# Two token mixings and the order of transposes at the start of a fused mixing and two-MLP kernel

## The reference

```
# x: (2, 4096, 192); weight_gen: (2, 4096, 8 heads, 7 taps); both MLPs: 192 -> 2048 -> 192
w = softmax(weight_gen, over the 7 taps)
mix[b, s, head, :] = sum over k of w[b, s, head, k] * x_pad[b, s + k, head, :]   # 24 features a head, 6 rows of zeros ahead
t = mix.reshape(8192, 192)
h = t @ moe_w_in;  t = max(0.01 * h, h) @ moe_w_out                      # MLP 1, leaky ReLU
h = t @ moe2_w_in; out = where(h > 0, h, exp(min(h, 0)) - 1) @ moe2_w_out  # MLP 2, ELU
```

## Time and profile before

| | us |
|---|---|
| median of 3 runs | 1184.88 |
| lowest and highest of them | 1182.89 and 1187.18 |
| the profiled execution | 1186.27 |
| span of its trace | 1183.6 |
| PE busy in the span | 1160.1 |
| DVE, ACT and POOL busy | 661.4, 750.1 and 422.3 |

### The profile page before, as it was taken

How to read it: one execution, slowest core, us unless ns; L and a number is a source line. 1 busy time by engine, 2 the same in 40 slices (tenths; PEclk the granted TensorE clock), 3 DMA queues, 4 the chain that set the end, 5 groups by cost and what they waited for, 6 DMA issues and landing times.

```text
span 1183.6 us, 22757 instructions
## 1 busy us (share of the span) xinstructions
PE 1160.1 (98%) x9808; PEld 927.1 (78%) x9808; DVE 661.4 (56%) x690; ACT 750.1 (63%) x846; POOL 422.3 (36%) x409
## 2 busy tenths in 40 slices
PE   6899999999999999999999999999999999999998
PEld 4777887878878777887878878778787878878776
DVE  6766736456474554636446374564736556364554
ACT  3566757567575665657666575665757657575665
POOL 5727531707135090541806226080440806200000
PEclk9999999999999999999999999999999999999999
DMA  5312021020101101021020110201121020110000
GB/s 171 115 50 67 25 78 28 28 79 22 57 28 47 59 28 52 28 78 28 28 66 27 65 28 28 79 28 52 28 78 28 28 65 22 34 28 28 15 28 27
DMA packets 44724, 55.45 MB, mean 47 GB/s; under 512 B 4117, under 2 KB 32915, under 8 KB 44625
## 3 DMA queue, kind: packets, MB, share of 16 engines
q1 hardware_dynamic: 44624, 54.01, 14.8%
HBM read 36.29 MB, written 17.69 MB: 46 GB/s over the span
## 4 chain that ended last, share of the span: by engine, by line
PE 87%; DVE 4%; ACT 3%; POOL 3%; issue 2%; DMA 1%; SPq 0%; POOLq 0%
PE y_a_rows L617 27%; PE hidden L549 27%; PE y_b L610 19%; PE hidden L553 9%; PE hidden L578 5%; DVE hid_lo L1125 2%; DVE act L1100 2%; ACT hid_hi L915 1%; ACT act L899 1%; POOL mix L325 1%; POOL prod L313 1%; DMA wk<-in_weight_gen_dram 0%; ACT ya L873 0%; DMA xw<-in_x_dram 0%; POOL prod L337 0%
## 5 line engine op out<-in xcount | busy, mean ns | idle before, releaser
L617 PE MATMUL y_a_rows<-hid_hi,dn 64*128 64x512 f32 x2048 | 574.7, 392 | 0.0
L610 PE MATMUL y_b<-hid_hi,dn 64*128 64x512 f32 x1024 | 401.5, 392 | 0.5 <-PE y_b L610 0.2
L610 PE MATMUL y_b<-hid_lo,dn 64*128 64x512 f32 x1024 | 400.9, 392 | 0.0
L617 PEld LDWEIGHTS y_a_rows<-hid_hi,dn 64*128 64x128 f32 x2048 | 332.5, 185 | 44.8
L617 PE MATMUL y_a_rows<-hid_lo,dn 64*128 64x512 f32 x1024 | 359.2, 391 | 0.0
L1125 DVE TENSOR_TENSOR hid_lo<-hidden,hid_hi 128x1024 fp32r<-128x1024 f32 x128 | 156.5, 1222 | 231.4 <-ACT hid_hi L915 231.2
L1125 DVE TENSOR_TENSOR hid_lo<-act,hid_hi 128x1024 fp32r<-128x1024 f32 x127 | 169.8, 1337 | 178.4 <-ACT hid_hi L915 176.7
L897 ACT ACTIVATE hidden<-hidden 128x1024 f32<-128x1024 f32 x127 | 128.2, 1009 | 184.5 <-PE hidden L553 184.5
L313 POOL TENSOR_TENSOR mix<-xw,wk 128x384 f32<-128x384 f32 x30 | 39.0, 1301 | 571.8 <-DVE wk L1041 566.3
L899 ACT ACTIVATE act<-hidden 128x1024 f32<-128x1024 f32 x127 | 130.3, 1026 | 141.7 <-PE hidden L553 135.3
L549 PE MATMUL hidden<-in_a_hi,up_a_hi 64*128 64x512 f32 x1020 | 205.5, 399 | 7.2 <-DVE act L1100 3.4
(11 more groups left out here) (104 smaller groups left out, 1189.4 us busy)
## 6 DMA issues: line engine op xcount, KB each, us to landing
xw<-in_x_dram SPq DMA_DIRECT2D x14, 960.0 KB
raw_b<-squares_out SPq DMA_DIRECT2D x60, 96.0 KB, 2.2
out_dram<-staged SPq DMA_DIRECT2D x15, 384.0 KB, 2.5
squares_in<-prod SPq DMA_DIRECT2D x56, 96.0 KB, 2.0
squares_out<-ya SPq DMA_DIRECT2D x15, 256.0 KB, 2.0
raw_a<-squares_in SPq DMA_DIRECT2D x14, 256.0 KB, 2.8
raw_d<-in_moe_w_out_dram SPq DMA_DIRECT2D x8, 384.0 KB, 3.4
raw_a<-in_moe_w_in_dram SPq DMA_DIRECT2D x8, 256.0 KB, 3.7
```

The source lines that it names most:

```text
L610: return nc.tensor.matmul(y_b[:, :], dn[m][rows, f, P:2 * P], v[rows, s % HB, HALF[i]], start=start, stop=stop)
L617: return nc.tensor.matmul(bank[:, :], dn[m][rows, f, first:first + P], v[rows, s % HB, HALF[i]], start=(f == 0 and n == 0), stop=(f == FT ...
```

## The change

**First mixing.** Two more buffers, `term4` and `term5`, are laid into the part of `act` that the first phases don't use. Products 4 and 5 go to them and product 6 to `staged_rows`, so that no product waits for PE, and `s_termu` is gone. On DVE the first part of chunk 1's softmax (`softmax_a(1)`) moves from ahead of the mixing to between the two parts of chunk 0's input; on ACT its exponential moves behind chunk 0's input.

**Warm-up.** The two matmuls of L789 are gone.

**Chunk 1's input.** Part 0 is turned behind step 7 of phase 0. Phase 1 begins with the down work of step 5, then part 1 is turned, then the down work of step 6; up of step 8 follows in both parts. Step 9 takes the down work of step 7, and step 10 is up alone. ACT and DVE split part 0 behind their work on step 7.

**Layout.** `wk1`, the softmax weight buffer of odd chunks (896 bytes a partition), is allocated last, so that every buffer between moves by its size.

```diff
@@ -94,7 +94,7 @@
         xw = sb("xw", [P, PAD + J, D], f32)
-        wk = [sb(f"wk{n}", [P, J * H, TAPS], f32) for n in (0, 1)]
+        wk = [sb("wk0", [P, J * H, TAPS], f32)]
         wmax = sb("wmax", [P, J * H], f32)
         wsum = sb("wsum", [P, J * H], f32)
         wrec = sb("wrec", [P, J * H], f32)
@@ -122,7 +122,10 @@
         ya = [sb(f"ya{m}", [P, T], f32) for m in (0, 1)]
         yb = [sb(f"yb{m}", [D2, T], f32) for m in (0, 1)]
         staged = sb("staged", [P, 2, 2 * D], f32)
+        wk.append(sb("wk1", [P, J * H, TAPS], f32))
         staged_rows = staged[:, :, :].rearrange("p a (j d) -> p (a j) d", j=J // 2)
+        spare = act[:, :, :].rearrange("p a n -> p (a n)")[:, T:T + 2 * J * D].rearrange("p (a j d) -> p a j d", a=2, j=J)
+        term4, term5 = spare[:, 0], spare[:, 1]
         hidden = ps("hidden", [P, 2, 2 * T])
         y_a = [ps(f"y_a_rows{h}", [P, T]) for h in (0, 1)]
@@ -152,7 +155,6 @@
         s_mul = sem("mix_steps")
         s_term = sem("first_mix_steps_gpsimd")
         s_termv = sem("first_mix_steps_vector")
-        s_termu = sem("first_mix_terms_summed")
         s_turna = sem("first_mix_128_features")
         s_mix = sem("mix_ready")
         s_mixt = sem("mix_transposed")
@@ -213,12 +215,11 @@
         assert TAPS == 7
-        FIRST_TERMS = ((prod, 1), (prod2, 2), (mix, 5), (prod, 10))
+        FIRST_TERMS = ((prod, 1), (prod2, 2), (mix, 5), (term4, 10))
         FIRST_STEPS = FIRST_TERMS[-1][1]
         MIX_STEPS = 2 * TAPS - 1
         EARLY = 2
-        WARM = 2
         J_POOL = 1
         QUARTERS = 4
         DN_PARTS = 4
@@ -346,21 +347,17 @@
             eng.wait_ge(done, 4)
             add(mix, staged_rows)
-
-            eng.wait_ge(s_termu, 1)
-            product(4, prod)
+            product(4, term4)
+            product(5, term5)
             eng.wait_ge(done, 5)
-            product(5, staged_rows)
-
-            eng.wait_ge(s_termu, 2)
-            product(6, prod2)
+            product(6, staged_rows)
             eng.wait_ge(done, 7)
-            add(prod, staged_rows)
+            add(term4, term5)
             eng.wait_ge(done, 9)
-            add(prod, prod2)
+            add(term4, staged_rows)
         def split_down(eng, ops, m, n):
@@ -704,7 +701,8 @@
                         last.then_inc(s_turna, 1)
                     for j in range(J):
                         last = nc.tensor.matmul(by_token(turn_b)[:, j], term[:, j, P:D], ident[:, :], start=False, stop=(end and j == J - 1))
-                    last.then_inc(s_mixt if end else s_termu, 1)
+                    if end:
+                        last.then_inc(s_mixt, 1)
             def transpose_mix(c, part):
@@ -735,11 +733,17 @@
                         up_first()
                         continue
                     of, step = (dm, ST - LAG + s) if s < LAG else (m, s - LAG)
-                    if known(ph) and ph == 1 and s == 0:
-
-                        pe.wait_ge(s_lo, g - LAG + 1)
-                        down_open(of, step, g - LAG)
-                        down_close(of, step, g - LAG)
+                    if ph == 1 and s == 0:
+
+                        pe.wait_ge(s_lo, g - 2)
+                        down_open(0, ST - 3, g - 3)
+                        down_close(0, ST - 3, g - 3)
+                        transpose_mix(1, 1)
+
+                        pe.wait_ge(*down_split(0, DN_PARTS - 1))
+                        pe.wait_ge(s_lo, g - 1)
+                        down_open(0, ST - 2, g - 2)
+                        down_close(0, ST - 2, g - 2)
                     if s == 0:
                         pe.wait_ge(s_min if m else s_xin, 2 * (c + 1))
@@ -757,7 +761,14 @@
                         pe.wait_ge(s_g, ST * c_two + (s - 2) % ST + 1)
                     up(m, input_of(m, c), g, s, False)
-                    if known(ph) and (ph == 0 and s < LAG or ph == 1 and s == 0):
+                    if ph == 0 and s < LAG or ph == 1 and s in (0, 2):
+                        up(m, input_of(m, c), g, s, True)
+                        continue
+                    if ph == 1 and s == 1:
+
+                        pe.wait_ge(s_lo, g - 1)
+                        down_open(0, ST - 1, g - 2)
+                        down_close(0, ST - 1, g - 2)
                         up(m, input_of(m, c), g, s, True)
                         continue
                     if known(ph) and ph in (0, 2) and s in (3, 5, 7):
@@ -766,9 +777,6 @@
                     if known(ph) and ph == 2 and s == 7:
                         pe.wait_ge(*down_split(1, DN_PARTS - 1))
-                    if known(ph) and ph == 1 and s == 1:
-
-                        pe.wait_ge(*down_split(0, DN_PARTS - 1))
                     pe.wait_ge(s_lo, g - LAG + 1)
                     down_open(of, step, g - LAG, ph if s == LAG and dm is not None else None)
@@ -779,14 +787,11 @@
                     else:
                         up(m, input_of(m, c), g, s, True)
                         down_close(of, step, g - LAG)
-                    if s in (6, 7) and known(ph) and ph == 0:
-                        transpose_mix(1, s - 6)
+                    if ph == 0 and s == 7:
+                        transpose_mix(1, 0)
             pe.wait_ge(s_id, 2)
             sum_first_mix()
-
-            for _ in range(WARM):
-                nc.tensor.matmul(y_a[0][:, 0:P], ident[:, :], ident[:, :], start=True, stop=True)
             run(pe, phase)
             for d in range(LAG - 1, 0, -1):
@@ -948,8 +953,8 @@
                     if known(ph) and g == END:
                         last_step()
                         continue
-                    if known(ph) and (ph, s) in ((0, 7), (1, 0)):
-                        mlp1_input_hi(1, ph)
+                    if (ph, s) == (1, 0):
+                        mlp1_input_hi(1, 1)
                     if s == LAG - 1 and dm is not None:
                         take_y(dm, dc, ph - 1)
                     activation(m, c, g, s)
@@ -961,6 +966,8 @@
                         if s:
                             rounding(1, c, g - 1, s - 1)
                         exponential(c, s)
+                    if (ph, s) == (0, 7):
+                        mlp1_input_hi(1, 0)
                     if m == 1 and s in (5, 6) and not (known(c) and c >= CH - 2):
                         mlp1_input_hi(c + 2, s - 5)
                     if m == 0 and s in (3, 4) and not (known(c) and c == 0):
@@ -982,11 +989,11 @@
                             round_down(1, DN2_AT.index((ph, s)))
             softmax_exp(0)
-            softmax_exp(1)
             round_up(0, 0)
             round_up(0, 1)
             mlp1_input_hi(0, 0)
             mlp1_input_hi(0, 1)
+            softmax_exp(1)
             round_down(0, 0)
             run(act_e, phase)
             take_y(1, CH - 1, LAST)
@@ -1133,8 +1140,8 @@
                     if known(ph) and g == END:
                         last_step()
                         continue
-                    if known(ph) and (ph, s) in ((0, 7), (1, 0)):
-                        mlp1_input_lo(1, ph)
+                    if (ph, s) == (1, 0):
+                        mlp1_input_lo(1, 1)
                     if s == LAG - 1 and dm is not None:
                         add_y(dm, dc, ph - 1)
                     if s == 0 and dm == 1:
@@ -1151,6 +1158,8 @@
                         softmax_b(2)
                     if m == 1 and s == 2 and not (known(c) and c >= CH - 2):
                         turn_mix(c + 2)
+                    if (ph, s) == (0, 7):
+                        mlp1_input_lo(1, 0)
                     if m == 1 and s in (5, 6) and not (known(c) and c >= CH - 2):
                         mlp1_input_lo(c + 2, s - 5)
                     if m == 1 and s == 3 and not (known(c) and c >= CH - 3):
@@ -1178,11 +1187,11 @@
             softmax_a(0)
             softmax_b(0)
-            softmax_a(1)
             mixing_share()
             split_up(0, 0)
             split_up(0, 1, (0,))
             mlp1_input_lo(0, 0)
+            softmax_a(1)
             mlp1_input_lo(0, 1)
             softmax_b(1)
             split_up(0, 1, (1,))
```

## The result

| | before | after |
|---|---|---|
| median, us (runs) | 1185.24 (4) | 1156.91 (4) |
| lowest to highest | 1182.89 to 1187.18 | 1156.57 to 1158.20 |
| span of the profiled execution | 1183.6 | 1154.9 |
| PE busy in the span | 1160.1 | 1133.8 |

The ratio is 0.9764 (95% interval 0.9744 to 0.9783): 2.4% or 28 us less. The forecast was 1179.5 us, 5.4 less, with a range down to 1177.0.

A forecast was written before the change was run, and what follows sets the result against it. PE, busy 98% of the span, was taken to bound the kernel. Phase 1's 4.6 us plus the start's 0.8 made 5.4, from the median 1184.88 to 1179.5 us; own range 1178.0 to 1181.2, over all 1177.0 to 1183.2.

The forecast's parts named there:

- Layout: costed at nothing: Every matmul slot on PE: moving the buffers changes nothing, slots stay 0.2335 us; term of 0.
- slower, by the layout: Rival, chance 0.04: moved buffers cost PE more in each of 4904 slots; at 2 ns a slot, 1189.3 us.
- Phase 1: Reordered steps around chunk 1's transposes: step 11 begins at 71.5 in place of 76.12, 4.6 us gained.
- wait for the mixing: Part 0's transposes behind step 7: mixing is there 1.2 us before they are reached, so no wait; the gap was 3.3 us.
- the tie of part 1's transposes: At 57.8 us, PE reaches part 1's transposes just as DVE finishes part 0's rest; no wait taken.
- slow clock at step 7: Step 7 took 6.18 us in place of 4.42 behind PE's gap; its loss of 1.75 us goes.
- the new wait of 1.0 us: PE ahead of up of step 11 waits for hid_lo of step 9, a loss of 1.0 us.
- steps take 4.4 us as before: Behind step 11, steps keep their length and POOL's next mixing moves forward with them.
- The start: First mixing ends at 18.65 in place of 19.76, 1.1 us; 0.8 us reaches PE, bounds 0 and 1.1.
- DVE and POOL exclude each other: Rival, chance 0.05: first mixing ends at 20.85, the start costs 1.1 us in place of giving 0.8; 1181.4 us.
- The clock: Rival, chance 0.11: without the warm-up matmuls the clock falls at the start, up to 1.75 us; 1181.2 us.
- The warm-up's removal: Two matmuls of 0.71 us at 21.92: PE still waits for DVE afterwards, so removing them is itself worth nothing.

The follow-up runs named there:

- e5: The kernel before with only the first mixing changed (own buffers for products 4 and 5, softmax_a(1) and its exponential behind): 1185.32 us, ratio 0.9981.
- e6: The changed kernel with the two warm-up matmuls put back ahead of step 0: 1156.48 us, ratio 0.9742.
- e1: The kernel before with one edit, wk1 allocated last (the new layout alone): 1165.64 us, ratio 0.9804.
- q5: The kernel before with a pad of 128 bytes a partition ahead of hid_hi alone: 1178.33 us, ratio 0.9897.

## Why the prediction was wrong

**The step that failed** is "Layout: costed at nothing, since slots of 0.2335 us hold for products that read quite different buffers". The term was 0; measured, the layout alone gives 2.0% (interval 1.7 to 2.2), 20 to 26 us. The rival "slower, by the layout" had the place and the unit right, some nanoseconds in each of 4900 slots, and said that the other sign was as possible; it got 0.04 and the other sign got nothing in the range. The reason that I gave against it was no evidence: the buffers that I compared are all laid at the same place modulo 256, as each is a multiple of 256 bytes long, and so are all weights. The rows had no contrast in the one thing that the edit changes. What the runs showed in place of the 0 is 5.3 ns less in each slot (0.2283 for 0.2335 us). With bounds from both sides for this term, as for every other unknown cost, the range would have been far wider.

**Phase 1: right up to step 11.** Forecast 4.6 us and step 11 at 71.5 in the frame of before; the transposes alone gave 71.35 and a gain of 5.1 us (3.1 to 7.1). No wait for the mixing, none at the tie of part 1's transposes, no slow clock at step 7, and the new wait of 1.0 us where it was put. That the lead is kept behind step 11 ("steps take 4.4 us as before") is borne out by the median alone; the one trace of the old layout with both reorderings has lost most of it, to waits for in_b and a slightly longer slot.

**The start: right in mechanism, too small.** Forecast: DVE's first product near 8.1, last add at 18.65, in_b's rest at 22.45, 0.8 us for PE. Measured in the changed kernel: 7.87, 18.19, 21.68, and step 0's product of in_b at 22.43 in place of 23.99, 1.6 us. Of the difference about 0.15 us is an earlier landing of x, and 0.3 comes from the ten operations, which took 10.3 us, 1.03 each, in place of 10.6. The last 0.3 is softmax_a(1): I let it hold in_b's rest up, but it fits into the time in which DVE waits for ACT (0.86 us at 23.25), so the lead of 1.57 us at the last add arrives whole. From the landing of x to step 0's product of in_b it takes 15.94 us before, 14.51 after and 14.49 in e5, so 1.4 us is what the edit gives.

**DVE and POOL exclude each other** fell: 1.03 us a pair for ten pairs, with both at work, against 1.28 by the sum of the lone times. By the rule of the Trainium skill (SBUF — State Buffer, Who interferes with whom) they would block each other for whole instructions; the trace shows each slowed beside the other, but less than that.

**The clock.** The warm-up's removal is worth nothing that can be told, as forecast. The granted clock is 1.00 in the windows from 13.5 to 1000 us. It is 0.52 from 10.3 to 13.5 us, during the first terms, which PE turns well ahead of the last add, so nothing waits for it. That stretch comes with the new first mixing and not with the missing warm-up: from 12.0 to 13.5 us the clock is 0.50 in e5 and e6, which have the new mixing and the warm-up, and 1.00 before and in e1, which have the old mixing.

**Together.** The kernel after without the layout is at 0.9934 (0.9910 to 0.9958), 7.8 us less, where the forecast of 5.4 lies inside. With the layout: 6.9 us ahead of step 11 and 21.8 behind it. Behind it, 1107.5 us of before (1183.6 - 76.12) times 5.3 / 233.5 are 25 us by estimate, of which 2.2 went into the longer waits for DVE's activation. The rest, about 1 us, was not traced. (The prediction's own range has a slip: 1178.0 to 1181.2 us is 3.7 to 6.9 us below its median, not 3.3 to 6.9. Nothing hangs on it.)

**What stays open.** Why the distance between the weights and the streamed buffers acts on the slot, and its form: 32, 64, 128 and 192 bytes have no order that these runs explain, and the mixed layout of q5 has a pattern of its own. Distances below 32, and other operand shapes, were not tried.

## What to carry to other kernels

An edit that moves buffers is an edit of every instruction that reads them. If PE bounds the kernel, compare the slot (busy time over pairs of matmuls) before anything else, and when an allocation changes, look at where the weights and the streamed buffers lie relative to each other modulo 256 bytes; a pad of 128 bytes ahead of the first streamed buffer gave this kernel 2.2% (1.9 to 2.6) with no other edit. And a row argues against an effect only if the rows compared differ in the thing that is changed.

## What the runs showed of the hardware

- A pair of 64-row matmuls of 512 columns at the 2.4 GHz level takes 0.2283 us with weights and streamed operand at the same place modulo 256 bytes, and 0.2302 (64 bytes apart) to 0.2349 (192 apart) otherwise, busy time over pairs in 400 us of steady work. From start to start it is 226.9 ns at best and 233.3 at worst. The Trainium skill (TensorE: Matmul & The Clock Gate, Part 1) gives N / 2.4 GHz and about 2.5 ns for one matmul of N columns, an estimate of 0.216 us for 512; no kernel here reaches that.
- A PE that is 2% faster met DVE's activation of MLP 2 earlier in each of 16 phases: 5.6 us of waits in place of 3.4.
- A DVE and a GpSimd tensor_tensor with all inputs in SBUF, side by side, took 1.03 us a pair over ten pairs of products and sums (changed kernel, 7.92 to 18.19 us), more than either alone (a product: 0.757 and 0.522 us) and less than their sum of 1.28.
